# First layer of block 0 in two sets of 256 tokens, each begun once its two batches are attended

## What is computed

```python
for t in range(S):                                   # S = 768
    cur = einsum('bhd,bhe->bhde', u * k[t], v[t])
    y[t] = einsum('bhd,bhde->bhe', r[t], state + cur)
    state = w[t][..., None] * state + einsum('bhd,bhe->bhde', k[t], v[t])
x = y.transpose(...).reshape(3072, 384)
x = (sigmoid(x @ w_gate) * (x @ w_val)) @ w_out      # 384 -> 1536 -> 384
x = x @ w2_in                                        # 384 -> 2048
out = where(x > 0, x, exp(min(x, 0)) - 1) @ w2_out   # 2048 -> 384
```

## Time and profile before

| | |
|---|---|
| times of three runs | 1202.12, 1203.12, 1210.94 us; median 1203.12 |
| the profiled execution, span | 1203.3 us |
| PE busy | 1155.1 us, 96% |
| DVE busy | 669.5 us, 56% |
| ACT busy | 472.2 us, 39% |
| POOL busy | 295.5 us, 25% |
| mean granted TensorE clock | 0.987 of 2.4 GHz |
| DMA share | 21.0% |

### The profile page before, as it was taken

How to read it: one execution, slowest core, us unless ns; L and a number is a source line. 1 busy time by engine, 2 the same in 40 slices (tenths; PEclk the granted TensorE clock), 3 DMA queues, 4 the chain that set the end, 5 groups by cost and what they waited for, 6 DMA issues and landing times.

```text
span 1203.3 us, 18133 instructions
## 1 busy us (share of the span) xinstructions
PE 1155.1 (96%) x6336; PEld 1006.2 (84%) x6336; DVE 669.5 (56%) x1044; ACT 472.2 (39%) x889; POOL 295.5 (25%) x290
## 2 busy tenths in 40 slices
PE   5778998999999999999999999999999999999999
PEld 4666777888888888888888888889999899899998
DVE  8777868494839393939393933354433334343433
ACT  2433444333333333333333333365544545454543
POOL 5563434143615351535153520000000000000000
PEclk9879998999999999999999999999999999999999
DMA  5451624122312231133204004220100101010000
GB/s 85 80 95 44 106 65 86 40 37 30 54 40 27 38 48 43 20 45 39 53 12 54 0 19 138 66 71 23 52 0 12 40 0 52 0 52 0 26 0 26
DMA packets 153413, 51.80 MB, mean 43 GB/s; under 512 B 126624, under 2 KB 148768, under 8 KB 153376
## 3 DMA queue, kind: packets, MB, share of 16 engines
q1 hardware_dynamic: 153376, 51.33, 21.0%
HBM read 41.88 MB, written 9.44 MB: 43 GB/s over the span
## 4 chain that ended last, share of the span: by engine, by line
PE 82%; DVE 11%; issue 4%; ACT 2%; DMA 0%; POOL 0%; DVEq 0%; SPq 0%; POOLq 0%; ACTq 0%
PE ps L606 21%; PE ps L639 17%; PE ps L631 16%; PE ps L615 10%; PE ps L544 7%; DVE RKW L828 6%; PE ps L560 3%; PE ps L534 3%; PE ps L565 2%; PE ps L573 2%; DVE hl L897 1%; DVE A L853 1%; DVE WS L917 1%; ACT RKW L669 1%; PE ps L581 1%
## 5 line engine op out<-in xcount | busy, mean ns | idle before, releaser
L606 PE MATMUL ps<-xh,WS 128*128 128x512 f32 x864 | 251.3, 408 | 1.6 <-DVE xl L888 1.6
L669 ACT ACTIVATE hh<-work 128x512 fp32r<-128x512 f32 x168 | 106.4, 633 | 287.5 <-DVE work L907 205.5
L544 PEld LDWEIGHTS ps<-RKW 128*128 128x128 f32 x1152 | 157.2, 203 | 59.1 <-DVE RKW L828 38.8
L544 PE MATMUL ps<-RKW 128*128 128x128 f32 x1152 | 167.6, 293 | 34.2 <-DVE RKW L828 34.0
L639 PE MATMUL ps<-WS,hh 128*128 128x384 f32 x768 | 198.0, 339 | 0.5 <-DVE hl L897 0.5
L828 DVE TENSOR_TENSOR RKW<-RKW,WL 64x256 f32<-64x256 f32 x288 | 186.1, 646 | 16.1 <-PE ps L544 13.7
L606 PEld LDWEIGHTS ps<-xh,WS 128*128 128x128 f32 x864 | 155.1, 190 | 30.7 <-issue 1.8
L897 DVE TENSOR_TENSOR hl<-work,hh 128x512 fp32r<-128x512 f32 x168 | 133.0, 791 | 85.3 <-ACT hh L669 84.3
L631 PE MATMUL ps<-xh,WS 128*128 128x512 f32 x576 | 164.2, 397 | 0.0
L615 PE MATMUL ps<-hh,WS 128*128 128x512 f32 x432 | 161.6, 411 | 0.4 <-DVE hl L897 0.3
L934 DVE SCALAR_TENSOR_TENSOR work<-work,ps 128x512 f32<-128x512 f32 x96 | 66.0, 688 | 172.2 <-ACT work L757 172.2
(11 more groups left out here) (67 smaller groups left out, 1324.7 us busy)
## 6 DMA issues: line engine op xcount, KB each, us to landing
nat<-in_w_dram SPq DMA_DIRECT2D x24, 192.0 KB, 3.7
nat<-in_k_dram SPq DMA_DIRECT2D x24, 192.0 KB, 4.8
nat<-in_r_dram SPq DMA_DIRECT2D x24, 192.0 KB, 5.2
V<-in_v_dram SPq DMA_DIRECT2D x24, 192.0 KB, 4.5
x_scratch<-work SPq DMA_DIRECT2D x6, 768.0 KB, 3.5
nat<-x_scratch SPq DMA_DIRECT2D x6, 768.0 KB, 5.2
out_dram<-Yt SPq DMA_DIRECT2D x5, 768.0 KB, 3.9
RKW<-in_moe_w_in_dram SPq DMA_DIRECT2D x16, 192.0 KB, 2.4
```

The costliest lines, as they stand in the source:

```text
L544: last = mm(bank[b][:, p * P:(p + 1) * P].rearrange("p (e i l) -> p e i l", e=2, l=L), K[:, g, :], Rb[:, :, :, 1, :], start=True, stop=True)
L606: last = mm(ps[:, VAL if val else GATE, :], gate_w(a, val, j, c), xp[b][:, c, :], start=(i == 0 and c == 0), stop=(i == 2 and c == KC - 1))
L669: return nc.scalar.activation(o, i, ACT.Copy)
```

## The change

The first layer of block 0 is done in two sets `m` = 0, 1 of 256 tokens, one for each half of the batches; the blocks 1 to 5 keep their 512 tokens (their sets are counted as n + 1). `cols(m)` gives the columns of set m.

- FIRST is now the 24 parts of half 0 of block 0 and a small XT (6 transposes, splits of 128x256).
- `HALVES` takes the place of mixed(0): the 108 thirds of set 0, then the 108 of set 1, every one now of 128x256 matmuls, with 73 attention parts spread over the first 207 of the 216: the 24 parts of half 1 of block 0, its XT, and the 48 parts of block 1. XT of block 1 and the last 6 thirds follow as before.
- The six early splits of weights stand at L5, L6 and KT of half 0 instead of from L3 on in half 1. The other 30 still follow one to a finished group of thirds, which are now half as wide.
- Eight weight pieces are loaded at once at the start: six raw buffers in `work` (two of them lie over `sig` and `h`) and two in the half of `Yt` that half 1 writes later. The gate's first sigmoid waits for their splits. One semaphore for each piece.
- Waits on counts (`s_att`, `a_x2`, `d_xlo`, `d_lo` and others) are shifted by what block 0 counts more.

The core of the diff:

```diff
-    PARTS = [("a", hf, name, b) for hf in range(HALF) for name in STAGES for b in range(U)]
+    PARTS = [[("a", hf, name, b) for name in STAGES for b in range(U)] for hf in range(HALF)]
+    def spread(dense, parts, room):
+        steps = []
+        for i, third in enumerate(dense):
+            steps.append(third)
+            steps += [parts[s] for s in range(len(parts)) if s * room // len(parts) == i]
+        return steps
-    FIRST = PARTS + [XT]
+    FIRST = [(0, *part) for part in PARTS[0]] + [(0, "a", 0, "XT", 0)]
+    HALVES = [(m, *third) for m in range(HALF) for third in THIRDS + LATE]
+    HALVES = spread(HALVES[:-len(LATE)],
+                    [(0, *part) for part in PARTS[1]] + [(0, "a", 1, "XT", 0)] + [(1, *part) for part in PARTS[0] + PARTS[1]],
+                    len(HALVES) - len(LATE) - 3) + [(1, *XT)] + HALVES[-len(LATE):]
-    EARLY = [len(FIRST) // 2 + 10 + 2 * x for x in range(AHEAD)]
+    EARLY = [FIRST.index((0, "a", 0, name, b)) for name in ("L5", "L6", "KT") for b in range(U)]
...
-        NR1 = 4
-        raw_w1 = work[:, 0:NR1 * KC * P].rearrange("p (n f) -> p n f", n=NR1)
+        NR1, ONCE = 4, 4
+        raw_w1 = work[:, 0:(NR1 + 2) * KC * P].rearrange("p (n f) -> p n f", n=NR1 + 2)
+        raw_w1_y = Yt[:, G:2 * G].rearrange("p (n q) e d -> p n (q e d)", n=2)
...
                     a, b = PASSES[i]
                     for c in range(KC):
-                        last = mm(ps[:, VAL if val else GATE, :], gate_w(a, val, j, c), xp[b][:, c, :],
+                        last = mm(ps[:, VAL if val else GATE, t], gate_w(a, val, j, c), xp[b][:, c, t],
                                   start=(i == 0 and c == 0), stop=(i == 2 and c == KC - 1))
...
             pe.wait_ge(p_const, 1)
-            for step in FIRST:
-                attention(0, *step[1:])
-            mixed(0)
+            for n, *step in FIRST + HALVES:
+                if step[0] == "a":
+                    attention(n, *step[1:])
+                else:
+                    layer1(n, *step)
             with pe.Fori(1, NB - 1) as i:
                 mixed(i)
```

More of the change, by code:

```diff
@@ L157, in build @@
         v_loaded = [sem(f"v_loaded{i}") for i in range(HALF)]
-        w1_loaded = [sem(f"w1_loaded{i}") for i in range(NR1)]
+        w1_loaded = [sem(f"w1_loaded{i}") for i in range(N1)]
         w2_loaded = [sem(f"w2_loaded{i}") for i in range(NR)]
@@ L496, in bank_free @@
             def bank_free(n, hf, name, i):
[L498 removed]
+                order = ORDER0 if isinstance(n, int) and n == 0 else ORDER
+                m = order.index((hf, name, i)) - NBK
                 if m < 0:
[L500 to L501 removed]
+                    if order is ORDER0:
                         return
[L503 removed]
+                    n = n - 1
+                    order = ORDER0 if isinstance(n, int) and n == 0 else ORDER
+                ph, pname, pi = order[m]
                 q = 2 * n + ph
@@ L576, in attention @@
                 else:
-                    pe.wait_ge(d_y, 4 * (n + 1))
+                    by_half = isinstance(n, int) and n == 0
+                    pe.wait_ge(d_y, 2 * (hf + 1) if by_half else 4 * (n + 1))
                     for c in range(KC):
                         bank_free(n, hf, name, c)
-                        for b in range(B):
+                        for b in range(hf * U, (hf + 1) * U) if by_half else range(B):
                             last = nc.tensor.transpose(bank[c][:, b * P:(b + 1) * P],
@@ L650, in mixed @@
                     else:
-                        layer1(i, *step)
+                        layer1(i + 1, *step)
             pe.wait_ge(p_const, 1)
-            for step in FIRST:
-                attention(0, *step[1:])
-            mixed(0)
+            for n, *step in FIRST + HALVES:
+                if step[0] == "a":
+                    attention(n, *step[1:])
+                else:
+                    layer1(n, *step)
             with pe.Fori(1, NB - 1) as i:
@@ L773, in _ @@
             nc.scalar.activation(first[:], ident[:, 0:1], ACT.Sigmoid)
-            for s, step in enumerate(FIRST):
-                attention(0, *step[1:])
-                if s in EARLY:
-                    split_w1(EARLY.index(s))
-            x = AHEAD
-            for step in MIXED:
+            x = 0
+            for s, (n, *step) in enumerate(FIRST + HALVES):
                 if step[0] == "a":
-                    attention(1, *step[1:])
+                    attention(n, *step[1:])
                 else:
-                    layer1(0, *step)
-                    if step[-1] == 2 and x < N1:
-                        split_w1(x)
-                        x += 1
+                    layer1(n, *step)
+                if s in EARLY or (step[0] != "a" and step[-1] == 2 and x < N1):
+                    split_w1(x)
+                    x += 1
             assert x == N1
@@ L955, in _ @@
             nc.vector.reduce_sum(odd[:], ident[:, 1:P:2], axis=AX.X).then_inc(d_zero, 1)
-            for s, step in enumerate(FIRST):
-                attention(0, *step[1:])
-                if s in EARLY:
-                    split_w1(EARLY.index(s))
-            x = AHEAD
-            for step in MIXED:
+            x = 0
+            for s, (n, *step) in enumerate(FIRST + HALVES):
                 if step[0] == "a":
-                    attention(1, *step[1:])
+                    attention(n, *step[1:])
                 else:
-                    layer1(0, *step)
-                    if step[-1] == 2 and x < N1:
-                        split_w1(x)
-                        x += 1
+                    layer1(n, *step)
+                if s in EARLY or (step[0] != "a" and step[-1] == 2 and x < N1):
+                    split_w1(x)
+                    x += 1
+            assert x == N1
             with dve.Fori(1, NB - 1) as i:
```

190 lines of the change are left out of this document (100 added, 90 removed).

## The result

| | before | after |
|---|---|---|
| times, median | 1203.12 us (1199.83 to 1210.94, 9 runs) | 1218.75 us (1210.85 to 1630.59, 9 runs) |
| span of the profiled execution | 1203.3 us | 1209.9 us |
| mean granted clock | 0.987 | 0.987 |

The ratio of the times is 1.0091, 95% interval 1.0058 to 1.0124: about 0.9% slower, where I had said 1199, 0.3% faster. (The 1630.59 is one disturbed run, left out of the ratio; the median of the other eight is 1217.4.

The account below looks back on a forecast made before the run. PE was taken to bound the last 973.3 us, so only the head, ending at 230.0, could move: 53.3 + 169.7 = 223.0, plus 3 for the clock, 226.0; 4 us less than 1203.12 gave 1199, range 1188 to 1210.

Parts of the forecast that it names:

- 256 columns at 0.117: Block 0's layer: a 256-column matmul takes 0.117 us, half of a 512-column one, so a third costs 0.352 us.
- The layer begins at 53.3: End of FIRST: 48.5 us, plus 2.2 for four splits, plus 2.5 for XT, with rounding.
- The stages: HALVES to the head's end: nine stages, each the larger of PE's and VectorE's need, sum to 169.7 us.
- far under is wrong: Sign in 53:226: PE's wait for r far under 20 us would mean the "PE stays fed" rival holds.
- The head ends at 226.0: Everything ahead of the steady loop: ends at 226.0 instead of 230.0, 4 us less.
- PE stays fed: Rival for the head: VectorE runs ahead, only two stages exceed PE's need, head ends at 213.8, time 1187; chance 0.16.
- weights come late: Rival in KT to XT: attention's loads hold the queue before the next weight, 2 to 4 us lost, 1203; chance 0.05.
- The last 973.3 us are PE's and stay as they are.: From 230.0 to 1203.3, PE sets the pace and the change leaves the time as it is.
- The clock term, 3 us (bounds 0 and 17): L stages of the head: 3 us charged for falls of the granted clock while PE waits for VectorE.
- 48.5 us without a clock term: FIRST: the time until the second half began, taken from the kernel before as the base of the layer's start.
- rival of the low clock: L stages: clock falls and stays low, 20 us instead of the 3 charged, 1216; chance 0.13.
- The range: Whole kernel: 1188 to 1210 us, leaving out half of the fed case and most of the two slow ones.

Follow-up runs that it names:

- 1.: The changed kernel with 64 more instructions (128 already satisfied semaphore waits) at the start of PE's list; median 1210.45 us, ratio 1.0037.
- four slow kernels: The changed kernel (1218.75 us), it with its loop moved by 256 instructions (1210.44), and the kernel before moved by 137, with waits (1224.17) or mostly transposes (1213.27).

## Why the prediction was wrong, by its steps

- *256 columns at 0.117.* Right: groups of three begin 0.35 to 0.36 apart, where nothing is waited for. Timeline of PE of after:

```profile
54.39 0.52 PE L642 MATMUL ps<-xl,WS 128*128 128x256 f32 x3
54.74 0.52 PE L642 MATMUL ps<-xh,WS 128*128 128x256 f32 x3
55.10 0.60 PE L568 MATMUL ps<-ident,nat 128*128 128x128 f32 x4
```

- *The layer begins at 53.3.* It began at 52.01, in the profile of the lower group.
- *The stages.* Forecast against measured: T 12 and 13.4, L 36 and 34.8, KT to XT 15.4 and 16.8, T 11 and 11.2, L 27 and 30.5, KT to S 13.9 and 14.1, T 9 and 9.3, L 26.5 and 25.6, the end 18.9 and 18.9. The sum came to 174.6 instead of 169.7; 3 us of that I had charged to the clock. The largest miss is the second L stage, 3.5 us, where the clock was 0.94. PE's wait for r from 53 to 226 is 17.1 us, somewhat under the 20 I had set as "far under is wrong".
- *The head ends at 226.0.* At 226.6, from the balance above: 3.4 us gained where 4.0 were forecast.
- *Rival "PE stays fed".* No: PE waited for r as forecast.
- *Rival "weights come late".* It happened once, where it was placed, and small. Attention's loads hold SP's queue from 92.93 to 101.69, the weights follow, and ScalarE waits. Timelines of SP and of ScalarE in after:

```profile
92.93 1.00 SPq L282 DMA_DIRECT2D nat<-in_w_dram  x2
...
97.98 3.71 SPq L308 DMA_DIRECT2D V<-in_v_dram  x2
101.73 0.88 SPq L318 DMA_DIRECT2D work<-in_moe_w_val_dram  x1
```
```profile
105.34 0.52 ACT L707 ACTIVATE WS<-work 128x384 fp32r<-128x384 f32 x1 [3.28 <-DMA work<-in_moe_w_val_dram]
```

  The longest wait of this kind in the profile of before is 0.3 us. The stage around it (KT to XT) was 1.4 us over its forecast, which bounds what this cost there. PE itself waits for a split once, 1.86 us at 127.48, in the T stage that was 0.2 over; whether the late load stands behind that wasn't tested. None of it was removed by an experiment, so its price stays open between 0 and some 3 us.
- *"The last 973.3 us are PE's and stay as they are."* **This step failed, and it alone turns the profiled execution from 3.4 us faster to 6.6 slower.** I had compared the work in the loop, which is the same, and not its place in PE's list. It cost 9.9 us, some 8.4 in gaps behind three jumps back and 1.5 in a fall of the clock behind one of them. The number needed was in reach: the change adds 324 matmuls and 324 weight loads ahead of the loop, and q8 has a row on the page of before. What I lacked was any row that shows a penalty, since before has none in its loop; it could have been a rival, not a term.
- *The clock term, 3 us (bounds 0 and 17).* Mis-sized for the median, and in the wrong place. In the profiled run the L stages had 0.86, 0.94 and 1.00, near what I charged. But what separates the upper group is a fall ahead of all of that, in KT to XT of half 0 in FIRST, 6.6 us, which I had carried over from before as 48.5 us without a clock term. Five of eight undisturbed runs of the changed kernel are in the upper group, and so its median is too. None of the five was profiled; the profile of a run in the upper group of 1. shows the fall. The mean granted clock of each run fits: in 1. 0.977 to 0.982 in the upper group and 0.986 or 0.987 in the lower; in the changed kernel 0.979 to 0.983 in four of the five and 0.984 to 0.987 in the lower group, but 0.987 in the run of 1216.10, whose time this doesn't explain. The kernel before has such times more rarely: one of 9 runs, then three of 23, four of 30 and none of 11 at 1210 to 1212. My rival of the low clock held that a busy PE brings the clock back; the profile of 1. has it at 0.50 from 44 to 60 with PE busy.
- *The range* 1188 to 1210 held neither group: 1199.3 + 9.9 + 0.6 is 1209.8, the span of the profiled run (its time is 1211.63), and the upper group lies 5 to 10 us above that, most of it a fall of the clock as far as is known.

## What to carry to other kernels

An edit ahead of a hardware loop also moves the loop in the engine's instruction list. If the loop's body is long (here 1568 instructions) look at "issue" gaps behind the jump back and at the instruction queue's packets per turn before you explain a loss by the work, and shift the loop by some instructions to test it. If a kernel's times fall into two groups, compare granted clocks stretch by stage between profiles of each group, ahead of the changed place too. And ask whether a cheaper edit at the true wait (here the order of two copies on ScalarE) gives what a new schedule is to give.

## What the runs showed of the hardware that I had not expected

- A loop of about 1568 PE instructions runs free of code loads in five placements tried and pays 2.3 to 4.6 us a turn, with 7 to 10 packets of 16 KB, in the one that all four slow kernels share (the place of before plus 137, modulo 256). The Trainium skill's "Advanced Engine Details and Errata", section "ISA Cache", adds "Only 2 cache lines!" to its figures. For PE the free placements speak against two, since the loop is longer than 512 instructions and has 1 or 0 packets a turn there behind the first turn. Where the slow stretch begins and ends between +32 and +169 wasn't tried.
- The gaps can cost more than themselves: behind 1.66 us of work in 4 the granted clock was 0.58 in the next 4 (473 to 481 of after), 1.5 us more in that turn.
- The loss can't be seen in the DMA share, and PE's busy time of a turn hardly shows it (share 0.25 in 469 to 595 with it and 0.25 in 226.6 to 347 without; busy 122.53 us in that turn, 120.68 in one of before).
- A satisfied semaphore wait on PE costs 0.11 us; 137 instructions of them moved the first transposes from 6.86 to 16.69.
- The clock stood at 0.50 for 16 us (44 to 60 in the profile of 1.) while PE was busy in nearly all of it (15.8 us, and 18.52 of the 20.00 us from 40) with matmuls of 48, 96 and 128 columns.
